# A mixture-of-experts tail on one core: expert loops written out, and GpSimd's gathers put ahead of its scatters

## The reference, cut to what matters

```python
skip_score = x @ w_skip
do_compute = skip_score > 0
out = x.copy()
xc = x[do_compute]
e_idx = np.argmax(xc @ w_gate, axis=1)
# gate_w: softmax probability of the chosen expert
for e in range(8):
    mask = e_idx == e
    h = np.maximum(xc[mask] @ w1[e], 0.0)         # 384 -> 1024
    y[mask] = gate_w[mask, None] * (h @ w2[e])    # 1024 -> 384
out[do_compute] = xc + y
```

## Time and profile before

| | |
|---|---|
| median of 3 runs | 895.24 us (892.25 to 895.81) |
| profiled execution, its own time | 895.62 us |
| its span | 893.9 us |
| mean granted clock of TensorE | 0.976 |
| PE busy | 774.3 us, 87% |
| DVE busy | 663.7 us, 74% |
| ACT busy | 495.5 us, 55% |
| GpSimd (POOL) busy | 416.3 us, 47% |

### The profile page before, as it was taken

How to read it: one execution, slowest core, us unless ns; L and a number is a source line. 1 busy time by engine, 2 the same in 40 slices (tenths; PEclk the granted TensorE clock), 3 DMA queues, 4 the chain that set the end, 5 groups by cost and what they waited for, 6 DMA issues and landing times.

```text
span 893.9 us, 27698 instructions
## 1 busy us (share of the span) xinstructions
PE 774.3 (87%) x10782; PEld 624.0 (70%) x10783; DVE 663.7 (74%) x1334; ACT 495.5 (55%) x1108; POOL 416.3 (47%) x498
## 2 busy tenths in 40 slices
PE   0123679999999999999999999999999899999985
PEld 0123558787777777777778788878777668778764
DVE  6485978888888888788888887866868873563382
ACT  5435555767576766666675766554464652441261
POOL 5213163627262635445453634352353665564473
PEclk9996599999999999999999999999999999999998
DMA  9489748577778777766768676347516765263100
GB/s 224 107 196 194 137 75 140 103 141 139 138 142 139 137 124 133 139 126 131 135 121 145 103 140 123 76 70 232 176 20 205 248 234 182 84 204 118 44 17 17
DMA packets 357277, 119.76 MB, mean 134 GB/s; under 512 B 330450, under 2 KB 348420, under 8 KB 356784
## 3 DMA queue, kind: packets, MB, share of 16 engines
q1 hardware_dynamic: 351424, 104.33, 55.9%
q0 software_dynamic: 3232, 7.64, 2.5%
q10 hardware_dynamic: 2512, 6.29, 2.0%
HBM read 63.53 MB, written 21.25 MB: 95 GB/s over the span
## 4 chain that ended last, share of the span: by engine, by line
PE 32%; DVE 24%; issue 11%; DMA 11%; ACT 11%; SPq 6%; POOL 4%; DVEq 0%; POOLq 0%; ACTq 0%
PE b_acc L849 8%; PE b_h L836 6%; PE b_h L743 6%; PE b_acc L756 6%; DVE stage L1485 4%; SPq L498 4%; DVE inv L1411 3%; DMA t_dram<-inv 3%; PE b_ch L682 3%; DVE inv L1417 3%; DMA natq<-x_dram,id_in 3%; ACT ga L954 2%; DMA operands<-t_dram 2%; ACT operands L954 2%; ACT stage L1074 2%
## 5 line engine op out<-in xcount | busy, mean ns | idle before, releaser
L1910 POOL TENSOR_TENSOR stage<-stage 128x256 f16<-128x256 f32 x192 | 142.7, 743 | 252.9 <-ACT stage L954 252.1
L743 PE MATMUL b_h<-stage,wt 128*128 128x256 f16 x1728 | 221.7, 274 | 11.2 <-DVE stage L1344 9.1
L756 PE MATMUL b_acc<-wt,stage 128*128 128x384 f16 x1152 | 218.4, 326 | 4.3 <-POOL stage L1910 3.4
L743 PEld LDWEIGHTS b_h<-stage,wt 128*128 128x128 f16 x1728 | 158.9, 98 | 31.6 <-DVE stage L1344 10.9
L756 PEld LDWEIGHTS b_acc<-wt,stage 128*128 128x128 f16 x1152 | 106.7, 97 | 59.1 <-POOL stage L1910 6.6
L954 ACT ACTIVATE stage<-stage 128x256 f16<-128x256 f32 x192 | 80.0, 417 | 106.4 <-DVE stage L1485 105.5
L1485 DVE SCALAR_TENSOR_TENSOR stage<-b_h,stage 128x256 f32<-128x256 f32 x192 | 80.8, 421 | 43.2 <-ACT stage L1074 41.6
L849 PE MATMUL b_acc<-wt,operands 128*128 128x384 f16 x552 | 97.3, 326 | 7.6 <-DVE operands L1525 7.6
L836 PEld LDWEIGHTS b_h<-y,wt 128*128 128x128 f16 x1656 | 93.5, 98 | 6.6 <-issue 4.7
L836 PE MATMUL b_h<-y,wt 128*128 128x128 f16 x1656 | 96.5, 219 | 1.6 <-DVE y L1344 0.7
L1417 DVE TENSOR_REDUCE inv<-inv 128x30 f32<-128x90 f32 (+4 forms) x180 | 85.1, 473 | 5.8
(11 more groups left out here) (215 smaller groups left out, 1292.9 us busy)
## 6 DMA issues: line engine op xcount, KB each, us to landing
operands<-in_moe_w_dram SPq DMA_DIRECT2D x18, 1536.0 KB, 7.5
a_sys<-a_dram SPq DMA_DIRECT2D x24, 256.0 KB, 4.3
kc<-operands SPq DMA_DIRECT2D x22, 256.0 KB, 4.1
natq<-in_q_dram SPq DMA_DIRECT2D x24, 192.0 KB, 3.9
raw_v<-in_v_dram SPq DMA_DIRECT2D x24, 192.0 KB, 4.2
stage<-y SPq DMA_DIRECT2D x96, 48.0 KB, 2.0
x_dram<-stage SPq DMA_DIRECT2D x24, 192.0 KB, 2.9
out_dram<-stage SPq DMA_DIRECT2D x24, 192.0 KB, 3.3
```

Of the source, the lines that this page charges most:

```text
L743: mm = pe.matmul(b_h[f % 2][:, 0:GT], wt[0][:, a, d * FF + f * P:d * FF + (f + 1) * P], xT[:, g % 2, b, d, :], start=(i == 0), stop=(i == ...
L756: mm = pe.matmul(b_acc[w][:, 0:DM], g16[:, f % 4, a, w * P:(w + 1) * P], wt[1][:, b, f * DM:(f + 1) * DM], start=(f == 0 and (a, b) == PAR ...
L1910: pool.tensor_tensor(g16[:, f % 4, LO, :], g32[:, f % 4, :], g16[:, f % 4, HI, :], ALU.subtract).then_inc(g_lo, 1)
```

## The change

GpSimd: the part of `tile_back` that keeps a tile (copy to `xg_keep`, the wait until the previous scatter has landed, `yo_left`) becomes `keep(t)`; the rest stays as `tile_back`. A turn of the loop is now `tile_next(t)`, `tile_back(t - 1)`, `keep(t)`, so that the copies of row t+1 and the gather of row t+2 come before the scatter of tile t-1, and the last scatter follows the loop.

DVE: `tile` now takes `tile_out(t - 1)` behind its quarter 0, and quarter 3 comes ahead of `tile_in(t + 1)`; quarters 1 and 2 come ahead of the two `hidden_low`. The last `tile_out` follows the last expert. In the written-out part only `tile_out(3)` goes away, since the first `tile` now does it.

ACT and DVE: all eight experts are written out, the last one without quarters. One register load per expert, that of the number of tiles of the next expert, stands behind the expert's first tile; the number of tiles before it is added up in registers. The places of the quarters on ACT stay.

```diff
-            def expert(e, q, last=None):
-                n = act.value_load(tile_n[0:1, 0, ds(e, 1)], min_val=1, max_val=NT)
-                before = act.value_load(tile_n[0:1, 1, ds(e, 1)], min_val=0, max_val=FIRST + MAXT)
+            def count(e):
+                return act.value_load(tile_n[0:1, 0, ds(e, 1)], min_val=1, max_val=NT)
...
+            QUARTERS = [((1, 1, 2, 3), None, (2, 0, 1, 0), (2, 0, 1, 1)), (None, (2, 0, 1, 2), None, (2, 0, 1, 3))]
+            QUARTERS += [[(e + 1, 1 - e % 2, e % 2, i) for i in range(4)] for e in range(2, E - 1)]
+            QUARTERS += [(None, None, None, None)]
+            n, before = count(0), FIRST
+            for e in range(E):
                 act.wait_ge(eh_done, 1 + 2 * before)
                 act.sem_inc(act_waited, 1)
...
+                tile(before, QUARTERS[e])
+                n_next, before_next = count(min(e + 1, E - 1)), before + n
                 with act.If(n > 1):
                     with act.Fori(1, n) as j:
                         tile(before + j)
...
+                n, before = n_next, before_next
```

```diff
@@ block.vector
             tile_in(FIRST)
-            tile_out(3)
             split_lo(1, 1, 2, 2)
...
                 if q[0]:
                     split_lo(*q[0])
-                hidden_low(t, 0)
+                tile_out(t - 1)
                 if q[1]:
                     split_lo(*q[1])
-                hidden_low(t, 1)
+                hidden_low(t, 0)
                 if q[2]:
                     split_lo(*q[2])
-                tile_in(t + 1)
-                tile_out(t)
+                hidden_low(t, 1)
                 if q[3]:
                     split_lo(*q[3])
...
+                tile_in(t + 1)
...
+            tile_out(before + (n - 1))
```

```diff
@@ block.gpsimd
-                pool.wait_ge(ids_ready, 1 if isinstance(t, int) and t == 1 else 2 * t - 2)
+                pool.wait_ge(ids_ready, t if isinstance(t, int) and t < 3 else 2 * t - 3)
...
-            def tile_back(t):
+            def keep(t):
                 pool.wait_ge(yo_ready, 1 + t)
                 waited()
                 pool.tensor_copy(xg_keep[:], tiles[:, ds(t % RING, 1), :].rearrange("p a m -> p (a m)")
                                  ).then_inc(xg_kept, 1)
                 pool.wait_ge(yo_scattered, 16 * t + 16)
                 pool.sem_inc(yo_left, 1)
...
+            def tile_back(t, ids_at):
                 pool.tensor_copy(id_out[:], ids[:, ds(t, 1)]).then_inc(ids_ready, 1)
+                pool.wait_ge(ids_ready, ids_at)
+                waited()
                 pool.wait_ge(yo_ready, 1 + t + 1)
-                waited()
-                pool.wait_ge(ids_ready, 2 * t + 3)
                 waited()
...
             with pool.Fori(FIRST, total) as t:
                 tile_next(t)
-                tile_back(t)
+                tile_back(t - 1, 2 * t + 2)
+                keep(t)
+            tile_back(total - 1, 2 * total + 1)
```

More of the change, by code:

```diff
@@ L1835, in tile, with count @@
                     split_lo(*q[0])
-                hidden_low(t, 0)
+                tile_out(t - 1)
                 if q[1]:
                     split_lo(*q[1])
-                hidden_low(t, 1)
+                hidden_low(t, 0)
                 if q[2]:
                     split_lo(*q[2])
-                tile_in(t + 1)
-                tile_out(t)
+                hidden_low(t, 1)
                 if q[3]:
                     split_lo(*q[3])
[L1847 to L1856, removed]
+                tile_in(t + 1)
+            def count(e):
+                return dve.value_load(tile_n[0:1, 0, ds(e, 1)], min_val=1, max_val=NT)
+            QUARTERS = [((1, 1, 2, 3), None, (2, 0, 1, 0), (2, 0, 1, 1)), (None, (2, 0, 1, 2), None, (2, 0, 1, 3))]
+            QUARTERS += [[(e + 1, 1 - e % 2, e % 2, i) for i in range(4)] for e in range(2, E - 1)]
+            QUARTERS += [(None, None, None, None)]
+            n, before = count(0), FIRST
+            for e in range(E):
+                tile(before, QUARTERS[e])
+                n_next, before_next = count(min(e + 1, E - 1)), before + n
                 with dve.If(n > 1):
@@ L1859, in expert @@
                         tile(before + j)
[L1861 to L1866, removed]
+                if e < E - 1:
+                    n, before = n_next, before_next
+            tile_out(before + (n - 1))
         @block.gpsimd
@@ L2050, in _ @@
                 tile_next(t)
-                if t == 0:
+                if t == 1:
                     pool.wait_ge(x2_stored, 64 * G)
                     waited()
-                tile_back(t)
+                if t:
+                    tile_back(t - 1, 2 * t + 2)
+                keep(t)
             pool.wait_ge(tiles_ready, 1)
```

## The result

| | before | after |
|---|---|---|
| median, us | 895.81 (5 runs, 892.25 to 896.93) | 931.21 (5 runs, 929.29 to 937.11) |
| ratio, 95% interval | 1 | 1.0416 (1.0376 to 1.0455) |
| profiled execution, us | 895.62 | 937.11, the longest of its five |
| its span, us | 893.9 | 935.4 |
| first tile to PE's last product, us | 215.81 | 250.55 |

A forecast was written before the change was run, and what follows sets the result against it. The prediction took PE, busy for 87% of the span, to bound the kernel, with POOL's order deciding the change. Its seven terms summed to +27.8 us on 895.6, making 923.4, against the median 923 us; range 903 to 942.

The forecast's parts named there:

- Tile 3: Term 1: tile 3's scatter waits behind row 4's gather and lands late, delaying `expert_down`; +5.5 us (+3.4 to +8).
- near 705: Sign that the forecast is right: `tile_out(2)` on DVE runs near 705 us instead of 699.3.
- Tiles 4 to 7: Term 2: PE goes at POOL's rate, three turns of 13.75 us and one of 10.55; +12.7 us (-2 to +24).
- Tiles 12 and 14: Term 3: each comes behind a tile of four splits with its load, turn 13.75 us; +5.1 us (0 to +11).
- Tiles 20 to 22: Term 4: two split tiles in a row, no load in flight, turn 11.55 us twice; +3 us (-1 to +6).
- Quiet tiles: Term 5: nine undisturbed tiles at POOL's 8.35 us for PE's 8.25; +1 us (0 to +13).
- that rival: POOL bounds every tile: quiet flight nearer 3.7 us, turn 9.75, 936 us, or 937 with low clock; chance 13%.
- Registers and VectorE's order: Term 6: one value load for two at expert starts, but two quarters and `tile_out` ahead of `hidden_low`; -0.5 us (-4 to +2).
- the ring: POOL's serial chain per tile: landing, copies, gather issue, scatter issue, landing; 8.35 us in an undisturbed turn.
- The clock: Term 7: stalls of 4 us and more in tiles 3 to 7 may lower PE's clock; +1 us (0 to +10).
- the 908 case: Rival: scatter flights stay quiet, 2.3 us, under weight loads too, giving 908 us; chance 22%.
- faster: Rival: earlier gather and copy take POOL's 18.4 us of waits off `tile_out`, giving 889 us; chance 10%.

The follow-up runs named there:

- written: Kernel before with all experts written out and one count fetched ahead, VectorE's and POOL's orders as before: 892.93 us, ratio 0.9970.
- pool_old: Changed kernel with POOL's part as before: 900.21 us, ratio 1.0077.
- out_first: Changed kernel with POOL's part as before and VectorE's `tile_out(t - 1)` ahead of quarter 0, quarters 0 and 1 each behind it or a `hidden_low`: 899.75 us, ratio 1.0049.
- moved_first: `moved` with POOL's first three tiles in the order of the kernel before: 902.66 us, ratio 1.0075.
- moved_peel: `moved_first` with the wait for scatter 2's landing put in tile 3's turn, ahead of row 5: 905.08 us, ratio 1.0094.
- best_b: `moved_first` with the landing wait between the next row's copies and its gather, and VectorE's quarters spread again: 899.48 us, ratio 1.0046.
- moved: Changed kernel with the landing wait and `yo_left` moved from `keep` to behind the next tile's copies and gather, from tile 3 on: 904.13 us, ratio 1.0101.
- small_after: Changed kernel with each weight load of experts 1 to 7 cut from 1.5 MB to 96 KB: 908.79 us.

## Why the prediction was right, step by step

The direction, the mechanism and its place were right, and 931.2 lies inside the range; the sum was 7.6 us short. It is nearer than its parts: terms 1 to 3 came out 11.7 us too low together, terms 4, 5 and 7 some 4.5 too high (what the clock cost is inside terms 1 to 3). By its terms:

1. *Tile 3*, +5.5 forecast, +7.5 measured. The chain was right almost to the row: `expert_down` was to start 5.9 us late and started 5.7 late (9.78 for 4.05), with a flight of 4.40 for 4.5; `tile_out(2)` at 710.50 is 704.9 on before's time (5.6 less), for "near 705". But the 4.5 stood for a flight beside a load, and with the loads cut this flight was still 4.01: the size was right, the reason wasn't, and so far the hit is luck. The other 2.1 us are the slow clock, 1.9 in the 12 products behind the wait and 0.3 in the transposes.
2. *Tiles 4 to 7*, +12.7 forecast, +15.2 measured (54.28 for 39.08). The scatters' issues follow each other by 14.2, 15.6, 11.8, 14.5 and 10.6 us, for 13.75 and 10.55. Of the 2.5 missing, 1.8 are again slow products, at the end of tile 7: 3.26, 0.84 and 2.39 us, for 2.11, 0.49 and 2.11 in quiet.
3. *Tiles 12 and 14*, +5.1 forecast, +12.3 measured, the step most off. Their flights were 6.5 us for the 4.5 that I took, which makes 4.1; two flights of the kernel before had shown as much (by their rows 7.0 and 5.5 us, not 6.9 and 5.4), and I had put them down as leaning high; slow products make 3.1 (3.74 and 3.60 for 2.11). Tile 13 gave 0.7 back.
4. *Tiles 20 to 22*, +3 forecast, +0.5 measured (28.80 for 28.29). No load flies there, as I said, and the slack took nearly all of it.
5. *Quiet tiles*, +1 forecast, 0 measured. The turn is 7.81 us, not 8.35: my 0.6 for the loop's end was already inside the 2.28 between the issue's end and the next copy. The flight of 2.3 was right, so POOL doesn't bound every tile, and that rival falls.
6. *Registers and VectorE's order*, -0.5 forecast. As a part of the whole it can't be read alone: `written` gains 0.4 us of stage and `pool_old` loses 7.1, but with POOL's new order VectorE's order makes no difference (250.44 and 250.55). I had missed that VectorE's order delays POOL when POOL is in its old order, by `out_first` not through quarter 0; in this change the ring covered it.
7. *The clock*, +1 forecast. By the three places above it was on the path for 1.8, 1.6 and 1.5 us at the ends of stalls, about 4.9 in all. In tile 3 it lengthened the tile too, but the next wait was shorter for it, since POOL's ring and not PE set when `tile_out(3)` went. This split is worked out from the rows; no run isolates the clock.

Not in the sum was the tail. `tile_out` and the scatter were to follow PE as before, at no cost. They follow it 1.15 us later (scatter issued 3.06 us after PE's last product for 1.91), because the last `tile_out` stands behind scatter 22's landing: it is the last row of DVE's timeline above, 2.29 us idle for `yo_left`.

The prediction took the inference of the Trainium skill (SBUF — State Buffer) on descriptor writing to mean that a gather's issue would stay at 1.05 us beside a split. That doesn't follow, since the issue also reads its indices from SBUF. The row of 2.29 us, which the sum went by, held.

The rivals: flights were not quiet beside loads (4.1 to 6.6 us), which ends the 908 case; and what it took for "faster", a flight near 1.2 and no blocked issues, was nowhere. What stays open is why a version with early gathers still loses some 8 us once in tiles 3 to 5; three more placements of the wait (`moved_first`, `moved_peel`, `best_b`) only moved the stall. That late gathers start it was read from rows, not tried by itself.

## What to carry to other kernels

On an engine that issues DMAs in order, a wait for a transfer's landing directly behind its own issue puts the flight into the engine's turn, and everything queued behind it goes at that rate. Here that was free in quiet tiles (7.81 us for PE's 8.25) and cost nearly all of the 35 us where turns took 11.8 to 15.6. Put work that doesn't need the landing in between; from `moved` to the changed kernel that alone is 26.1 us. Before moving one step ahead of another, write the turn as a sum, issue, flight, copies, and the next issue, for quiet and for loaded stretches, and look for the loss where the loaded sum is over the bounding engine's time per tile.

Time each part of such a change by itself. Here the one part that gained (0.3%) was hidden in a loss of 4%, and so was the 7.1 us that VectorE's order costs as soon as POOL has its old one.

## What the runs showed of the hardware

- In the changed kernel's trace the same scatter of 128 rows took 2.28 or 2.29 us from the end of its issue to the row copy waiting on it in quiet turns (2.18 and 2.19 in two of them, and 1.77 to the index copy ahead of the last scatter), and 4.1 to 6.6 us beside 1.5 MB weight loads. In `small_after`, with loads of 96 KB, two flights were still 4.01 and 3.23, so a load isn't all that makes one long. The Trainium skill (DMA: Bandwidth & Descriptors, Anatomy of one DMA) gives a fixed part and one by bytes, by which an estimate for its 197 KB is 2.45 us. The quiet turns are near that when counted from the issue's end (from its start they are 3.3); for a flight beside loads the measured 4.1 to 6.6 decide.
- In the routed stage of that trace every POOL instruction that began inside a DVE split ended only behind it, DMA issues too, nine of them 0.91 to 0.93 us behind the split's end: the gather's issue 2.27 and 2.29 us for 1.05, a scatter's 2.12 and 2.33 for 1.03, the ring copy 2.04 for 0.51. The Trainium skill (SBUF — State Buffer) infers that descriptor writing isn't held by such a DVE instruction, and says that reads from SBUF are. The issue as a whole was held here; since it takes its indices from SBUF (`id_in`), no run tells which of the two held it.
- PE's granted clock can fall and come back within a tile. Behind a wait of 3.81 us 12 products took 3.81 us for 2.11, which is nearly the lower of its two levels, 1.2 for 2.4 GHz; behind the wait of 5.60 us in tile 3 they took 4.00 at a granted clock of 0.50, and the next 12 were at 2.11 and 1.00 again.
